# Outputs of each duo taken stream by stream, the moved unit from the first stream, the moves ahead of a weight load, and the first up products in turns

## The reference

```python
for t in range(S):
    cur = np.einsum('bhd,bhe->bhde', u[None] * kt, vt)
    y[:, :, t] = np.einsum('bhd,bhde->bhe', rt, state + cur)
    state = wt[:, :, :, None] * state + np.einsum('bhd,bhe->bhde', kt, vt)
x = y as (B * S, H * D)                      # 3072 x 384
x = ((x @ w_a) * (x @ w_b)) @ w_out          # d_ff = 1536
h = x @ w_in2                                # d_ff = 2048
out = (max(h, 0) + alpha * min(h, 0)) @ w_out2
```

## Time and profile before

| | us |
|---|---|
| median of 3 runs | 1033.6 (1032.6 to 1034.42) |
| the profiled execution, its own time | 1033.08 |
| its span, first to last instruction | 1030.9 |
| PE busy | 1003.5 (97%) |
| PE, share of the chain that ended last | 94% |

### The profile page before, as it was taken

How to read it: one execution, slowest core, us unless ns; L and a number is a source line. 1 busy time by engine, 2 the same in 40 slices (tenths; PEclk the granted TensorE clock), 3 DMA queues, 4 the chain that set the end, 5 groups by cost and what they waited for, 6 DMA issues and landing times.

```text
span 1030.9 us, 29060 instructions
## 1 busy us (share of the span) xinstructions
PE 1003.5 (97%) x12448; PEld 978.7 (95%) x12448; DVE 561.0 (54%) x1170; ACT 288.1 (28%) x604; POOL 32.8 (3%) x29
## 2 busy tenths in 40 slices
PE   5699999999999999999999999999999999999998
PEld 4699999999999999999999999999999999999998
DVE  6566575664655646646542446645555545555454
ACT  3424413224133232241222333222222222222211
POOL 4600010000000000000000000000000000000000
PEclk9899999999999999999999999999999999999999
DMA  7453231301312113011020223010101010101000
GB/s 182 106 152 103 58 102 30 90 25 30 89 52 60 33 52 91 3 52 37 26 59 1 85 85 94 30 47 1 47 1 46 2 46 0 46 0 46 3 22 24
DMA packets 42167, 53.01 MB, mean 51 GB/s; under 512 B 5184, under 2 KB 42048, under 8 KB 42048
## 3 DMA queue, kind: packets, MB, share of 16 engines
q1 hardware_dynamic: 40624, 51.04, 17.5%
q10 hardware_dynamic: 1424, 0.23, 0.2%
HBM read 39.46 MB, written 9.44 MB: 47 GB/s over the span
## 4 chain that ended last, share of the span: by engine, by line
PE 94%; DVE 2%; issue 2%; DMA 1%; ACT 1%; SPq 0%; DVEq 0%; ACTq 0%
PE products L162 17%; PE products L163 16%; PE products L164 16%; PE acc L162 11%; PE acc L164 11%; PE acc L163 11%; PE products L676 6%; PE products L720 1%; PE products L691 1%; PE products L653 1%; PE products L733 1%; PE products L705 1%; DMA w_v<-in_w_dram 1%; DVE f_y L851 0%; DVE state L916 0%
## 5 line engine op out<-in xcount | busy, mean ns | idle before, releaser
L162 PE MATMUL products<-x_parts,weights_hi 128*128 128x384 f32 x576 | 202.0, 351 | 4.3 <-issue 3.1
L163 PE MATMUL products<-x_parts,weights_hi 128*128 128x384 f32 x576 | 195.2, 339 | 0.0
L164 PE MATMUL products<-x_parts,weights_lo 128*128 128x384 f32 x576 | 194.9, 338 | 0.0
L1161 DVE TENSOR_SCALAR leaky_low<-products,leaky_al 128x384 f32<-128x384 f32 x128 | 79.0, 617 | 169.5 <-PE products L164 169.4
L1021 DVE TENSOR_TENSOR g_sb<-a_g,products 128x384 f32<-128x384 f32 x96 | 53.2, 554 | 198.8 <-issue 140.2
L1108 ACT ACTIVATE leaky_g_hi<-leaky_g_sb 128x384 fp32r<-128x384 f32 x128 | 67.3, 526 | 295.0 <-DVE leaky_g_sb L1166 295.0
L499 ACT ACTIVATE g_hi<-g_sb 128x384 fp32r<-128x384 f32 x96 | 50.3, 524 | 251.8 <-DVE g_sb L1021 251.8
L162 PEld LDWEIGHTS products<-x_parts,weights_hi 128*128 128x128 f32 x576 | 108.9, 189 | 8.4 <-issue 5.1
L164 PEld LDWEIGHTS products<-x_parts,weights_lo 128*128 128x128 f32 x576 | 109.1, 189 | 0.0
L163 PEld LDWEIGHTS products<-x_parts,weights_hi 128*128 128x128 f32 x576 | 109.1, 189 | 0.0
L162 PE MATMUL acc<-g_hi,weights_hi 128*128 128x384 f32 x288 | 97.8, 340 | 2.0 <-DVE g_lo L1027 1.2
(11 more groups left out here) (83 smaller groups left out, 1763.5 us busy)
## 6 DMA issues: line engine op xcount, KB each, us to landing
k_in<-in_k_dram SPq DMA_DIRECT2D x16, 336.0 KB, 4.2
r_in<-in_r_dram SPq DMA_DIRECT2D x16, 336.0 KB, 5.3
stage<-in_w_out_dram SPq DMA_DIRECT2D x14, 384.0 KB, 3.4
w_v<-in_v_dram SPq DMA_DIRECT2D x16, 288.0 KB, 4.4
y_dram<-x_in SPq DMA_DIRECT2D x8, 576.0 KB, 4.4
x_in<-y_dram SPq DMA_DIRECT2D x8, 576.0 KB, 4.6
out_dram<-leaky_out_sb SPq DMA_DIRECT2D x7, 576.0 KB, 3.3
stage<-in_w_dram SPq DMA_DIRECT2D x10, 336.0 KB, 3.9
```

The costliest lines, as they stand in the source:

```text
L162: pe.matmul(out, w_hi, x_hi, start=first, stop=False)
L163: pe.matmul(out, w_hi, x_lo, start=False, stop=False)
L164: return pe.matmul(out, w_lo, x_hi, start=False, stop=last)
L1161: dve.tensor_scalar(self.low[f % 2][:, :], h, 0.0, self.al[:, f:f + 1], ALU.min, ALU.mult).then_inc(self.low_ready, 1)
```

## The change

- **PE, phase 10.** `state_products` is done for one stream at a time. In duo 0 the first stream's go ahead of `weighted_values(n, 1)`; in later duos the half that is not crossed does, and the crossed half comes behind.
- **Outputs.** ACT and DVE take stream 0 first. The moved unit is the first of stream 0, kept in the first half of `f_y`; it fills the blocks in the order 0, 1, 2. The rows of w_a and w_b are laid out to match.
- **Moves.** One semaphore for each block (`moved[q]`). For duo 0 SP issues both halves of block 0 and the first half of blocks 1 and 2; ACT issues the second halves.
- **Loads.** SP loads by `LOAD_AT`: piece 6 now comes at step 11, behind the moves and the loads of w.
- **First up products.** Both products of block 0 are taken together, one channel block after the other, and each channel block waits for its own outputs and moves alone.
- **Leaf products of duo 1.** Stream 1's go to `acc` instead of `products`, so they wait for no output; stream 0's wait for stream 0's outputs alone. `down(0)` waits until they are merged.

```diff
+LOAD_AT = [7, 8, 9, 11, 11, 11]
 X_LOAD, X_SPLIT = 4, 8
-OUTPUTS, MOVES = 6, 6
+OUTPUTS = 6
...
-            row0, last = 64 * block, D * (7 - block)
-            parts.append((row0, D, 0, [[2 * P, 2]] + dims, columns[0:2 * E2, :].rearrange("(k r) n -> r k n", k=2)[D * block:D * (block + 1)]))
-            parts.append((row0, D, 4 * P, dims, columns[D * (5 - block):D * (6 - block), :]))
+            row0, last = 64 * block, D * (2 + block)
+            parts.append((row0, D, 0, dims, columns[D * block:D * (block + 1), :]))
+            parts.append((row0, D, 2 * P, [[2 * P, 2]] + dims,
+                          columns[2 * E2:4 * E2, :].rearrange("(k r) n -> r k n", k=2)[D * (1 - block):D * (2 - block)]))
...
+            def leaf_ps(n, j, hd):
+
+                return (acc[hd], 0) if n == 1 and j == 1 else (products, stream_bank(j, hd))
...
-                last_hi, last_lo = f_y[:, S:S + TT].bitcast(F32R), f_y[:, S + TT:2 * S].bitcast(F32R)
-                units_of_0 = (0, 2, hi[0:ROWS, 0:2 * TT], lo[0:ROWS, 0:2 * TT])
-                units_of_1 = ((1, 1, last_hi, last_lo), (0, 1, hi[0:ROWS, 2 * TT:3 * TT], lo[0:ROWS, 2 * TT:3 * TT]))
+                moved_hi, moved_lo = f_y[:, 0:TT].bitcast(F32R), f_y[:, TT:S].bitcast(F32R)
+                units_of_0 = ((1, 1, moved_hi, moved_lo), (0, 1, hi[0:ROWS, 0:TT], lo[0:ROWS, 0:TT]))
+                units_of_1 = (0, 2, hi[0:ROWS, TT:3 * TT], lo[0:ROWS, TT:3 * TT])
                 parts = []
-                for j, par, group in ((1, 0, units_of_1), (1, 1, units_of_1), (0, 0, (units_of_0,)), (0, 1, (units_of_0,))):
+                for j, par, group in ((0, 0, units_of_0), (0, 1, units_of_0), (1, 0, (units_of_1,)), (1, 1, (units_of_1,))):
...
-                engine.dma_start(to, f_y[row0 + 16 * q:row0 + 16 * q + 16, S:2 * S].rearrange("p (h t) -> p h t", h=2)).then_inc(moved, 16)
+                engine.dma_start(to, f_y[row0 + 16 * q:row0 + 16 * q + 16, 0:S].rearrange("p (h t) -> p h t", h=2)).then_inc(moved[q], 16)
...
-                    for q in ((2, 0, 1) if n > 0 else (2, 0)):
-                        part = 3 if q == 2 else OUTPUTS - 1
+                    for q in range(KT):
+                        part = 3 if q == 0 else OUTPUTS - 1
                         sp.wait_ge(copied, outputs_copied(n, part))
                         sp.wait_ge(lowered, outputs_lowered(n, part))
-                        for row0 in (0, 64):
+                        for row0 in ((0, 64) if n > 0 or q == 0 else (0,)):
...
-                    for piece in early_at(LO_AT, step):
+                    for piece in early_at(LOAD_AT, step):
...
-                            act.wait_ge(lowered, OUTPUTS)
-                            for row0 in (0, 64):
-                                move_rows(act, n, 1, row0)
+                            act.wait_ge(lowered, outputs_lowered(n, OUTPUTS - 1))
+                            for q in range(1, KT):
+                                move_rows(act, n, q, 64)
...
-                    if n > 0:
-                        pe.wait_ge(copied, outputs_copied(n - 1, OUTPUTS - 1 if j == 0 else 3))
-                        pe.wait_ge(lowered, outputs_lowered(n - 1, OUTPUTS - 1 if j == 0 else 3))
+                    if n > 1 or (n == 1 and j == 0):
+                        pe.wait_ge(copied, outputs_copied(n - 1, OUTPUTS - 1 if j == 1 else 3))
+                        pe.wait_ge(lowered, outputs_lowered(n - 1, OUTPUTS - 1 if j == 1 else 3))
...
-                def state_products(n, crossed):
-
-                    last = [None, None]
+                def state_products(n, j, crossed):
+
+                    if crossed:
+                        pe.wait_ge(products_done[j], after(n, 8))
                     for c in range(CH):
-                        for j in range(2):
-                            for hd in range(2):
-                                par = 1 - hd if crossed else hd
-                                b = 2 * HALF * (n % 2) + 2 * (c % HALF) + par
-                                if b > 0:
-                                    last[j] = pe.matmul(view(products, stream_bank(j, par) + BLOCK * c, [[1, BLOCK]], D, 64 * (hd ^ j)),
-                                                        view(state[j], D * (BLOCKS * (c // HALF) + b), [[1, D]], D, 64 * hd),
-                                                        key_blocks(queries_of(n, j), hd, c, par),
-                                                        start=False, stop=True, skip_group_check=True)
+                        for hd in range(2):
+                            par = 1 - hd if crossed else hd
+                            b = 2 * HALF * (n % 2) + 2 * (c % HALF) + par
+                            if b > 0:
+                                last = pe.matmul(view(products, stream_bank(j, par) + BLOCK * c, [[1, BLOCK]], D, 64 * (hd ^ j)),
+                                                 view(state[j], D * (BLOCKS * (c // HALF) + b), [[1, D]], D, 64 * hd),
+                                                 key_blocks(queries_of(n, j), hd, c, par),
+                                                 start=False, stop=True, skip_group_check=True)
                     if crossed:
-                        last[0].then_inc(products_done[0], 1)
-                        last[1].then_inc(products_done[1], 1)
+                        last.then_inc(products_done[j], 1)
 
                 def outputs(n):
 
-                    for j in range(2):
-                        pe.wait_ge(r_stepped[j], 6 * n + 6)
-                    state_products(n, False)
-                    for j in range(2):
-                        pe.wait_ge(products_done[j], after(n, 8))
-                    state_products(n, True)
+                    pe.wait_ge(r_stepped[0], 6 * n + 6)
+                    state_products(n, 0, False)
+                    if n == 0:
+                        state_products(n, 0, True)
+                        weighted_values(n, 1)
+                    else:
+                        weighted_values(n, 1)
+                        state_products(n, 0, True)
+                    pe.wait_ge(r_stepped[1], 6 * n + 6)
+                    state_products(n, 1, False)
+                    state_products(n, 1, True)
...
+                def wait_x(tile, kt):
+
+                    part = 3 if kt == 0 else OUTPUTS - 1
+                    pe.wait_ge(copied, outputs_copied(tile, part))
+                    pe.wait_ge(lowered, outputs_lowered(tile, part))
+                    pe.wait_ge(moved[kt], 32 * (tile + 1))
+
+                def first_ups():
+
+                    shared.wait_piece(pe, shared.number["w_b", 0])
+                    for kt in range(KT):
+                        wait_x(0, kt)
+                        product_a = up_part(0, "w_a", a_ps, kt)
+                        if kt == KT - 1:
+                            product_a.then_inc(a_done, 1)
+                        else:
+                            pe.wait_ge(merged, merges(1, 0, 0))
+                        product_b = up_part(0, "w_b", b_ps(0), kt)
+                    product_b.then_inc(b_done, 1)
...
+                    if g == 0:
+                        pe.wait_ge(merged, merges(1, 0, 3))
```

44 lines of the change are left out of this document (27 added, 17 removed).

## The result

The changed kernel takes 1036.85 us (median of 8 runs, 1036.0 to 1039.2), the kernel before in the same series 1032.51 (8 runs, 1031.54 to 1034.42). The ratio is 1.0042, with the interval 1.0032 to 1.0053. The prediction said 1030.5 with a range up to 1032.6, so it was wrong in sign. The profiled execution has a span of 1037.2 us where before had 1030.9.

A forecast was written before the change was run, and what follows sets the result against it. From 56 us on PE's list at its pace bounds the kernel, with duo 0's start of g_lo of block 0 setting everything behind. Gain 3.5 less 0.4 added is 3.1 us: 1030.5 against the median 1033.6, range 1028.6 to 1032.6.

The forecast's parts named there:

- What is added: Phase 10 of duos 1 to 7: more runs and finer waits in PE's list cost 0.4 us (0 to 1.0).
- rival (d): Phase 10, duos 1 to 7: one stream uses two array quarters; if entries doubled, 8.7 us more, 1039.2; chance 0.07.
- The outputs: Duo 0: first output copy at 41.3 us instead of 42.89, last lowering at 43.95 instead of 45.56.
- The moves: Duo 0: SP issues moves from 43.05 us, four taking 2.8; first up product at 46.2 instead of 51.48.
- the slow bound: Duo 0: first up products end at 52.0 us if the clock is slow throughout, 49.5 if fast, instead of 56.81.
- What is late next: Duo 0: piece 6 lands at 52.9 to 53.75 us; ACT's split of it holds g_hi; gain 3.5 us.
- X: Start of g_lo of block 0 on DVE, 58.21 us before the change, predicted at 54.2 to 55.1.
- the first term: Duo 0: the gain from starting g_lo of block 0 earlier, 3.1 to 4.0 us, taken as 3.5.
- Rival (a): The clock falls in the new wait ahead of `down(1)`, costing 1.7 us: 1032.2; chance 0.13.
- Rival (b): Duo 0: piece 6 isn't late, first up products bind; gain 4.8 us or more, 1028.8 or less; chance 0.07.
- Rival (c): The gain is swallowed by another fixed-time wait behind, such as that at 98 us: 1033.4; chance 0.05.

The follow-up runs named there:

- e7: The changed kernel with 24 of 48 stationary columns in the state products of duos 1 to 7; one execution, 1040.54 us.
- e5: e1 with the mixed state products of duos 1 to 7 ordered row half by row half, both streams inside; one execution, 1031.29 us.
- e1: The changed kernel with both streams' state products mixed again in duos 1 to 7, as before the change; 1031.18 us, ratio 0.998.
- e3: e1 with ACT's g_hi of block 0 put ahead of the split of piece 6; 1027.89 us, ratio 0.9945.
- e8: e14's kernel with duo 0's state products mixed too, behind stream 1's weighted values; 1030.56 us, ratio 0.9982.
- e14: The same kernel as e3, run again in a later series; 1027.77 us, ratio 0.9953.
- e4: The changed kernel with 32 of 64 moving columns in the state products of duos 1 to 7; one execution, 1034.75 us.
- e6: e1 with the state products of duos 1 to 7 in runs of four of one stream, then four of the other; one execution, 1031.93 us.
- e11: e1 with the state products of duos 1 to 7 quarter by quarter, 12 entries in a row on each; one execution, 1045.91 us.
- e15: e1 with 32 of 64 moving columns in the mixed state products of duos 1 to 7; one execution, 1028.96 us.
- e12: e3 with duo 0's stream 0 states and stream 1 values by turns, and e5's order in duos 1 to 7; 1029.89 us, ratio 0.9975.

## Why the prediction was wrong

The sum was 3.5 - 0.4. Both terms failed, the second by far.

**What is added: 0.4 us said, 7.3 measured.** This is rival (d), which had 0.07 and the price 8.7. Its mechanism, place and price were right, as far as the runs show them: a quarter has a pace of its own, but that the load of weights stands in series in it is not shown (e7 halved their columns and the pace stayed). 624 entries at 14 ns more are 8.7; the traces show 7.3, 0.2 us a duo less, which the overlap of state products with the weighted values may save; it was not separated. The step that failed is the sentence that spoke against it, "each product is two entries on the same quarter already, and they keep 14 ns". 14 ns was the pace of all four quarters together; on its own quarter an entry had 56 ns, and a product's two entries 112. The earlier trace rows held that number: 96 entries in 1.45 us are 24 on each of four quarters, 60 ns each. Nothing in the trace said that a quarter could go faster, and the prediction should have asked for a row in which it did; it used a mean over four as if it were one's. In the Trainium skill, TensorEngine Tiling (Array Packing), Key Properties, tiles work independently and in parallel; the runs agree (one quarter 56 ns, two 28, four 14), and this was the sentence to follow. The other one, in the Trainium skill, TensorE: Matmul & The Clock Gate, The mechanism, lets a weight load overlap running matmuls only when the row group differs. The runs do not agree with it as a rule for the pace: e5 keeps the row group for two products and loses nothing (2.16 us), and the changed kernel changes it with every product and its entries take double (27 ns for 14).

**The outputs.** The holes in front of stream 1's values and of the leaf products closed as said. The first copy started at 42.65 for 41.3 and the last lowering ended at 46.9 for 44. This execution ran late from its start (first weighted values at 38.79, before at 37.01), which is 1.8 us of either and more than the whole of the first. The other 1.1 us of the second are the same error again: stream 0's 40 entries of state products took 1.8 us instead of 1.08, and stream 1's 1.9.

**The moves.** They began at 44.44 for 43.05, and four took 3.83 us for 2.8. Not for a slow issue: none took over 748 ns. The second ended at 45.83 and the third began at 47.00, just behind the last lowering of stream 1 (46.92), for which the prediction had 43.95. That wait of 1.2 us is for the most part the slower pace of the state products again. In e1 and e3, where the clock rose 3 to 4 us earlier, the four took 2.88 and 2.75 us. A slow issue like that of before did come in e8 and e14 (1.5 and 1.2 us), so striking it was luck here. The first up product started at 47.86 for 46.2, with a second wait of 0.4 us; the next block's up product started at 52.0, the slow bound, but at the full clock: it was the late begin that brought it there.

**What is late next.** The mechanism was right, with ScalarE's split of piece 6 waiting for its transfer and g_hi behind it. The size was off: 55.59, and 53.3 as the middle of the forecast; of these 2.3 us some 1.4 are the late begin of the moves and 1.0 their wait for stream 1. Then 1.29 us to X, as said: 56.88, a gain of 1.3 in this execution. e1, whose levels began 0.3 us earlier than before's, has X at 55.60, a gain of 2.6. Its series gains 2.1 us, so the first term by itself was 2.1 to 2.6 and not 3.5. The chain from X to g_lo of block 1 was 6.96 us, to the digit.

**Rival (a), the clock,** came as well, in the profiled execution: 0.50 from 58.4 to 65.2, worth 0.9 us by block 2 (1.7 said). It followed a wait of 2.09 us ahead of `down(0)`, a wait that the prediction had named (1.9). Of seven other executions with these waits the clock fell behind them in two, e4 and e5, where the longest wait was 2.3 us; where it was 1.8 (e1, e6, e7, e11, e15) it stayed full there. With the split behind g_hi the wait was 0.5 to 0.8, and in eight executions the clock did not fall behind it. It still can fall earlier: in e3, e11, e12 and e15 it was 0.50 for 3.4 to 6.8 us from a point between 47.6 and 49.7 on, among the first up products, with a wait of 2.5 to 3.3 us for the moves ahead of them. **Rival (b)** did not occur: where the split stood ahead of g_hi and the load behind the moves, ScalarE waited for piece 6 in every run. **Rival (c)** did not occur; e1's gain lasts from block 2 (2.6 us) to the end (1.8 us) with a loss of 0.8 in small waits.

With 3.5 in the first term and 7.3 in the second the sum would have been slower by 3.8 us; with 2.4 and 7.3 by 4.9. The medians say 4.3; neither sum has the 1.05 us between 130 and 139 us.

## What to carry to other kernels

Where small matmuls share the array as these do, count entries for each quarter: the time is the fullest quarter's count times its own pace, and a mean over mixed quarters is a fraction of that pace, never the price of one. Order work by stream only where the engine would stand idle anyway (here duo 0, 3 us gained), and keep the streams mixed where it is the bound (duos 1 to 7, 7 us lost). When a load is pushed back in a queue, look at what its consumer holds up on an engine that works in order: one copy put ahead of the waiting split was worth another 3 us.

## What the runs showed of the hardware

A 64x64 quarter of the array took an entry of an fp32 product (48 rows by 64 moving columns) every 56 ns at 2.4 GHz and every 107 ns at 1.2 GHz, and with 32 moving columns every 45 ns; 24 stationary columns instead of 48 left the pace as it was. If the time goes evenly with the moving columns, 34 of the 56 ns (an estimate, 56 less twice 11) go with neither number of columns; only two widths were run, and what the rest is stays open.

The 107 ns are from duo 0, where the views print a granted clock of 1.00 that is not a record: the first record of a full clock in the changed kernel's trace stands at 44.73 us, and there, within one run of state products, the pace turns from 107 to 56 ns. I take the stretch ahead of it for the lower level.

The quarters do not wait for each other in the order of the list. Runs of eight entries on two quarters cost 0.04 us in a phase of 144, runs of 12 on one cost 2.75, and runs of 24 or more on two 1.16; in the changed kernel the first value of stream 1 started with six state entries, listed ahead of it, still to start (113.84 in its rows). I had not expected either. The part ahead of the prediction says that all engines run their lists in order; for PE these runs show that it does not hold.
